# Gated attention and two MLPs on one core: outputs taken transposed, in strips of 32 columns

## What is computed

```python
for t in range(S):                      # a = (a_re, a_im) with its magnitude clamped
    new_re = ar * S_re - ai * S_im
    new_im = ar * S_im + ai * S_re
    kv = np.einsum('bhd,bhe->bhde', k[:, :, t], v[:, :, t])
    S_re, S_im = (new_re + kv, new_im)
    y[:, :, t] = np.einsum('bhd,bhde->bhe', q[:, :, t], S_re)
x = y.transpose(0, 2, 1, 3).reshape(B * S, H * D)      # 3072 x 384
h = x @ w_in;  g = elu(h);  x2 = g @ w_out             # 384 -> 2048 -> 384
out = maximum(x2 @ w1, x2 @ w2, x2 @ w3) @ moe2_w_out  # 384 -> 768 -> 384
```

## Time and profile before

| what | value |
|---|---|
| median of three executions | 1057.25 us (1054.79 to 1057.42) |
| the profiled execution | 1057.7 us, of which the span from the first to the last instruction is 1056.0 us |
| PE busy | 988.4 us, 94% of the span |
| DVE, ACT, POOL busy | 549.1, 439.4, 352.6 us |

### The profile page before, as it was taken

One profiled execution on the slowest core, in us unless ns is written; L12 is line 12 of the kernel. 1 busy time (PEld: TensorE's weight loads), 2 busy tenths in 40 slices (PEclk: granted clock), 3 DMA queues, 4 the chain that ended last, 5 costly groups with the idle time before them and its releaser, 6 DMA issues.

```text
span 1056.0 us, 14734 instructions
## 1 busy us (share of the span) xinstructions
PE 988.4 (94%) x5764; PEld 859.3 (81%) x5764; DVE 549.1 (52%) x720; ACT 439.4 (42%) x669; POOL 352.6 (33%) x277
## 2 busy tenths in 40 slices
PE   3767989989999999999999999999999999999997
PEld 1656879887888888888888788888789898888887
DVE  5888857575868677676858554235331212111110
ACT  5684536354646373736363533234321111212121
POOL 4346432233333343433433322135451212212110
PEclk9778988898999999999999999999999999999999
DMA  6311020202020201011010100140301010100000
GB/s 223 150 46 60 2 76 2 75 1 76 31 76 2 75 32 45 31 46 61 31 46 31 45 17 1 50 175 1 104 1 60 1 60 1 60 8 23 16 16 30
DMA packets 16301, 49.80 MB, mean 47 GB/s; under 512 B 2388, under 2 KB 5460, under 8 KB 15720
## 3 DMA queue, kind: packets, MB, share of 16 engines
q1 hardware_dynamic: 16232, 48.86, 13.4%
HBM read 39.35 MB, written 9.47 MB: 46 GB/s over the span
## 4 chain that ended last, share of the span: by engine, by line
PE 78%; DVE 7%; issue 6%; ACT 3%; POOL 2%; POOLq 0%; DVEq 0%; ACTq 0%
PE bank L997 75%; PE bank L1027 3%; DVE ge L755 1%; DVE t L758 1%; DVE t L780 1%; ACT ge L529 1%; PE bank L1079 1%; POOL hl L418 1%; DVE wil L761 1%; DVE qp L761 1%; DVE ge L758 0%; DVE kp L761 0%; DVE sc L761 0%; DVE xl L761 0%; POOL xl L418 0%
## 5 line engine op out<-in xcount | busy, mean ns | idle before, releaser
L418 POOL TENSOR_TENSOR gl<-ge,gh 128x512 fp32r<-128x512 f32 x96 | 131.4, 1369 | 317.9 <-ACT gh L529 317.9
L761 DVE TENSOR_TENSOR hm<-bank,hm 128x512 f32<-128x512 f32 x72 | 49.8, 692 | 226.6 <-PE bank L997 224.7
L529 ACT ACTIVATE ge<-bank 128x512 f32<-128x512 f32 x96 | 57.1, 595 | 209.5 <-PE bank L997 209.3
L997 PE MATMUL bank<-xh,wih 128*128 128x512 f32 (+1 forms) x336 | 132.4, 394 | 9.4 <-DVE xl L761 9.4
L755 DVE TENSOR_SCALAR ge<-ge 128x512 f32<-128x512 f32 x96 | 55.8, 581 | 157.8 <-ACT ge L529 155.8
L997 PE MATMUL bank<-gh,woh 128*128 128x512 f32 (+1 forms) x336 | 132.1, 393 | 0.7 <-POOL gl L418 0.7
L997 PE MATMUL bank<-xl,wah 128*128 128x512 f32 x324 | 126.3, 390 | 0.0
L997 PE MATMUL bank<-xh,wal 128*128 128x512 f32 x324 | 126.3, 390 | 0.0
L997 PE MATMUL bank<-xh,wah 128*128 128x512 f32 x324 | 126.2, 390 | 0.0
L997 PE MATMUL bank<-xh,wil 128*128 128x512 f32 (+1 forms) x336 | 126.0, 375 | 0.0
L997 PE MATMUL bank<-xl,wih 128*128 128x512 f32 (+1 forms) x336 | 125.7, 374 | 0.0
(11 more groups left out here) (99 smaller groups left out, 2009.9 us busy)
## 6 DMA issues: line engine op xcount, KB each, us to landing
ar<-in_a_re SPq DMA_DIRECT2D x12, 384.0 KB, 3.2
ai<-in_a_im SPq DMA_DIRECT2D x12, 384.0 KB, 3.8
qd<-in_q SPq DMA_DIRECT2D x12, 384.0 KB, 3.7
kd<-in_k SPq DMA_DIRECT2D x12, 384.0 KB, 3.1
vv<-in_v SPq DMA_DIRECT2D x12, 384.0 KB, 3.1
x_rows<-x2s SPq DMA_DIRECT2D x6, 768.0 KB, 3.3
x2r<-x_rows SPq DMA_DIRECT2D x6, 768.0 KB, 6.9
out_x<-osb SPq DMA_DIRECT2D x24, 192.0 KB, 1.9
```

Of the source, the lines that this page charges most:

```text
L418: return nc.gpsimd.tensor_tensor(dst, whole, high.bitcast(f32), ALU.subtract)
L529: return nc.scalar.activation(dst, src, f, **kw)
L761: return nc.vector.tensor_tensor(dst, a, b, op)
L997: return nc.tensor.matmul(dst, lhsT, rhs, start=start, stop=stop)
```

## The change

**Outputs.** `outputs(n)` now does all eight heads in one piece, and makes y transposed, features on partitions. Stationary are 32 columns of the values (or of the state), moving are the 128 columns of the masked scores (or of the transposed q), and the result goes to 32 PSUM partitions. The 384 features are twelve blocks of 32: for each head 32 of its 48 dimensions alone, and the remaining 16 of an even and an odd head together in one block, summed in PSUM with zeros in the gap. That makes 16 products with the scores and, from the second chunk on, 16 more with the state. Four products in a row go to the four strips of 32 partitions.

**What goes.** `y_columns`, `y_rows` and the tile `ysb`; `x_high` and `x_low` read the bank that `outputs` filled. Two pieces fewer take a turn of the three banks (y0, y1, x become y).

**What is laid out anew.** `vv` and `st` have 112 columns for each pair of heads (48, a gap of 16, 48) in place of 96. `increment` writes 64 and 48 columns in turn, `state_add` handles 448 columns in place of 384, and `state_decayed` is two operations on half the heads each. The rows of w_in are permuted on the host in the order of the features.

**The tables.** The last high and low parts of a unit pair stand at place 21, the increment at 22 and the state's addition at 23, so the boundary between tiles (`X_DONE`) comes two places earlier.

```diff
-        vv = sb("vv", [P, PAIR, W], f32, s1)
+        vv = sb("vv", [P, PAIR, H // 2, DP], f32, s1)
...
-        st = sb("st", [D2, B, W], f32, s1)
-        ysb = sb("ysb", [P, W], f32, s1)
+        st = sb("st", [D2, B, H // 2, DP], f32, s1)
...
-        PIECES = [f"{z}_{e}" for z in ("tq", "tk", "s", "lam", "phi", "y0", "y1", "x", "inc") for e in "ab"] + ["halves"]
+        PIECES = [f"{z}_{e}" for z in ("tq", "tk", "s", "lam", "phi", "y", "inc") for e in "ab"] + ["halves"]
...
-            def y_rows(n, half):
-                cols = slice(half * W // 2, (half + 1) * W // 2)
-                src, done = filled(act, f"y{half}", n)
-                if n >= 1:
-                    filled(act, "x", n - 1)
-                func(ysb[:, cols], src[:, cols], ACT.Copy).then_inc(done, 1)
...
-                src, _ = filled(act, "x", n)
+                src, _ = filled(act, "y", n)
...
-                tt(heads(st[:, b, :]), heads(st[:, b, :]), decay[:, b, :].unsqueeze(2).to_broadcast([D2, H, D]),
+                by_pair = decay[:, b, :].rearrange("p (j z) -> p j z", z=2)
+                tt(st[:, b, :, 0:D], st[:, b, :, 0:D], by_pair[:, :, 0:1].to_broadcast([D2, H // 2, D]), ALU.mult)
+                tt(st[:, b, :, DS:DP], st[:, b, :, DS:DP], by_pair[:, :, 1:2].to_broadcast([D2, H // 2, D]),
                    ALU.mult).then_inc(std, 1)
...
-            def outputs(n, half):
+            def outputs(n):
                 e, b, c = n % 2, batch(n), chunk_of(n)
...
-                for h in range(HB * half, HB * half + HB):
-                    cols = slice(h * D, (h + 1) * D)
-                    last = mm(dst[:, cols], sc[:, h, :], vv[:, e, cols], True, c == 0)
-                    if c >= 1:
-                        last = mm(dst[:, cols], qt[:, e, h, :], st[:, b, cols], False, True)
-                last.then_inc(done, 1)
-
-            def y_columns(n):
-                emptied(pe, "y0", n)
-                emptied(pe, "y1", n)
-                dst, done = filling(pe, "x", n)
-                for kk in range(KC):
-                    last = nc.tensor.transpose(dst[:, kk * P:(kk + 1) * P], ysb[:, kk * P:(kk + 1) * P], ident[:, :])
+                emptied(pe, "s0", n)
+                emptied(pe, "s1", n)
+                dst, done = filling(pe, "y", n)
+                state = st[:, b].rearrange("p j d -> p (j d)")
+                for kk, odd, begin, first_, last_ in ((0, 0, 0, True, True), (2, 1, DS + 16, True, True),
+                                                      (1, 0, 32, True, False), (1, 1, D, False, True)):
+                    for old in range(2 if c >= 1 else 1):
+                        for j in range(H // 2):
+                            h = 2 * j + odd
+                            cols = slice(j * DP + begin, j * DP + begin + 32)
+                            start, stop = first_ and old == 0, last_ and (old == 1 or c == 0)
+                            out_ = dst[32 * j:32 * j + 32, kk * P:(kk + 1) * P]
+                            if old:
+                                last = mm(out_, state[:, cols], qt[:, e, h, :], start, stop)
+                            else:
+                                last = mm(out_, values(e)[:, cols], sc[:, h, :], start, stop)
                 last.then_inc(done, 1)
...
-        "x_a": 15, "x_b": 23, "x_high_a": 16, "x_high_b": 23, "x_low_a": 16, "x_low_b": 23,
+        "state_add_b": 23, "x_high_a": 14, "x_high_b": 21, "x_low_a": 14, "x_low_b": 21,
```

More of the change, by code:

```diff
@@ L23, in build @@
     D = 48
+    DS = 64
+    DP = DS + D
     H = W // D
+    WP = H // 2 * DP
     D2 = 2 * D
@@ new lines, in build @@
+        "angle": -8, "halves": -9, "lam_a": -8, "lam_b": -8, "phi_a": -6, "phi_b": -5, "total": -8, "decays_a": -7,
+        "decays_b": -7, "decayed_a": -8, "decayed_b": -6, "reduced_a": -6, "reduced_b": -5, "sines": -4, "rotate_q_a": -3,
+        "rotate_k_a": 0, "rotate_q_b": 3, "rotate_k_b": 7, "tq_a": 1, "tq_b": 6, "tk_a": 2, "tk_b": 12, "s_a": 4, "s_b": 14,
+        "q_evac_a": 1, "q_evac_b": 7, "k_evac_a": 3, "k_evac_b": 12, "masked_a": 4, "masked_b": 15, "state_decay": -3,
+        "state_decayed_a": 6, "state_decayed_b": 12, "y_a": 11, "y_b": 19, "inc_a": 14, "inc_b": 22, "state_add_a": 15,
@@ L59, in build @@
+        "state_add_b": 23, "x_high_a": 14, "x_high_b": 21, "x_low_a": 14, "x_low_b": 21,
     }
     AT_FIRST = {
[L62 removed]
+        "square": -21, "square_im": -21, "squared": -20, "root": -18, "denominator": -17, "ln_first": -17, "ln_second": -15,
         "reciprocal_a": -15, "clamp": -16, "log_decay": -16, "reciprocal_b": -14, "negative": -13, "tangent": -11,
[L64 removed]
+        "arctan": -10, "angle": -9, "halves": -12, "lam_a": -14, "lam_b": -14, "phi_a": -9, "phi_b": -8, "total": -7,
@@ L284, in heads, with pairs @@
             return t.rearrange("p (h d) -> p h d", d=D)
+        def pairs(t):
+            return t.rearrange("p (j d) -> p j d", d=DP)
         def of_set(n):
@@ L366, in _ @@
                     both_parts(u + 1)
[L368 removed]
+            emptied(sp, "y", 2 * NU - 1)
             for n, w in enumerate((w1, w2, w3)):
@@ L1054, in increment, with values @@
                 for h in range(H):
-                    cols = slice(h * D, (h + 1) * D)
-                    last = mm(dst[0:D2, cols], kp[:, e, h].rearrange("p z d -> p (z d)"), vv[:, e, cols], True, True)
+                    cols = slice(h // 2 * DP, h // 2 * DP + DS) if h % 2 == 0 else slice(h // 2 * DP + DS, h // 2 * DP + DP)
+                    last = mm(dst[0:D2, cols], kp[:, e, h].rearrange("p z d -> p (z d)"), values(e)[:, cols], True, True)
                 last.then_inc(done, 1)
-            def outputs(n, half):
+            def values(e):
+                return vv[:, e].rearrange("p j d -> p (j d)")
@@ L1142, in attention @@
                     phase(PAIR * at(x, "phi_b") + 1)
-                if now("y0_a"):
-                    outputs(PAIR * at(x, "y0_a"), 0)
-                if now("y0_b"):
-                    outputs(PAIR * at(x, "y0_b") + 1, 0)
-                if now("y1_a"):
-                    outputs(PAIR * at(x, "y1_a"), 1)
-                if now("y1_b"):
-                    outputs(PAIR * at(x, "y1_b") + 1, 1)
-                if now("x_a"):
-                    y_columns(PAIR * at(x, "x_a"))
-                if now("x_b"):
-                    y_columns(PAIR * at(x, "x_b") + 1)
+                if now("y_a"):
+                    outputs(PAIR * at(x, "y_a"))
+                if now("y_b"):
+                    outputs(PAIR * at(x, "y_b") + 1)
                 if now("inc_a"):
@@ L1234 @@
             a = a.reshape(b, h, s // 128, 128, d).transpose(2, 3, 0, 1, 4).reshape(s // 128, 128, b, h * d)
+        if name == "v":
+            a = a.reshape(*a.shape[:3], h // 2, 2, d)
+            gap = np.zeros((*a.shape[:4], 16), a.dtype)
+            a = np.concatenate([a[..., 0, :], gap, a[..., 1, 32:], a[..., 1, :32]], axis=4).reshape(*a.shape[:3], -1)
         if name == "moe_w_in":
+            f = np.arange(h * d).reshape(h // 2, 2, d)
+            rows = [f[:, 0, :32], np.concatenate([f[:, 0, 32:], f[:, 1, 32:]], axis=1), f[:, 1, :32]]
+            a = a[np.concatenate([z.reshape(-1) for z in rows])]
             a = a.reshape(a.shape[0] // 128, 128, -1, 512).transpose(1, 2, 0, 3)
```

59 lines of the change are left out of this document (19 added, 40 removed).

## The result

The changed kernel is slower: 1094.3 us median of four executions (1090.99 to 1096.11), against 1056.63 us of the kernel before beside it. The ratio is 1.036, with a 95% interval from 1.033 to 1.039. The forecast was 1034 us, faster, with a range up to 1070. Both the sign and the range were wrong.

A forecast was written before the change was run, and what follows sets the result against it. PE's stream was taken as the bound from some 250 us on, DVE up to some 100 us. Terms +5.4 + 0.9 - 9.4 - 12 - 8 = -23.1 us from 1057.7, less 0.45, gave 1034 us; range 1015 to 1070.

The forecast's parts named there:

- DVE, ACT, POOL, SP: Work of these engines: ACT loses 48 copies, a third of their time is free after 250 us; 0 us.
- the chain of one full record for each product: In y, in-order starts let only half of each product overlap: 32 x 107 ns = 3.42 us, about 3.5 with fill.
- The products of y: y in PE's stream: 3.67 us a step against 3.40, +5.4 us; first chunk 1.93 against 1.71, +0.9 us.
- The lower end: Fastest y if all records overlap as far as they can be issued: 64 x 48 ns = 3.07 us.
- Entering the strips: PE's switch to another arrangement of the array ahead of y: 0.17 us, charged once a step.
- The transposes, -9.4 us: Each step loses the transposes ahead of `half_sums` and one more stop of PE: 24 x 0.39 us, -9.4 us.
- The tile boundary, -12 us: At tile boundaries PE's waits for `xl` and the half clock behind them go, 1 us left in all: -12 us.
- The first quarter, -8 us: PE's 6.6 us of early waits for a bank freed by the state's addition go: -8 us, ends 0 and -16.
- the waits move: Rival: boundary and first quarter give nothing, as another piece is late on the three banks; 1054 us, chance 0.09.
- The rival that the strips themselves bring the clock down: Each steady y is followed by 3.4 us of half clock, 1.7 us a step: +34 us, 1068 us, chance 0.07.
- Serial strips: Rival: the strips of y run one after the other, 7.02 us a step; 1104 us, chance 0.20.
- the exposed load: Rival: a product's load can't begin before the preceding matmul starts; y 4.3 to 5.1 us, 1048 to 1064 us, chance 0.12.

The follow-up runs named there:

- e1_early_copies: The changed kernel with the high and low copies of each later unit's first step at place 12, ahead of ACT's sines; 1017.81 us, ratio 0.961 to before.
- e8_q_copy_alone: e1_early_copies with ACT's copy of the second q at place 6, not 7, and the second unit's last high and low copies at 21, not 22; 1010.83 us.
- e7: e1_early_copies with each product of y cut into two of 64 moving columns; 1015.47 us in one execution.
- e3: The kernel before, with ACT's copy of the second half of each unit's first y one place later, behind the sines; 1108.53 us in one execution.
- e2: e1_early_copies with the products of y ordered strip by strip, finishing one strip before the next; 1095.27 us in one execution.
- e4: e1_early_copies with the first unit's first high and low copies at place 6, not 7 and 8; 1019.98 us, ratio 0.965 to before.

## Why the prediction was wrong

Two steps failed, and in opposite directions. The one that turned the sign is the term "DVE, ACT, POOL, SP: nothing": the copy that frees y's bank stood behind ACT's sines, which cost 76.5 us. The other is the chain of one full record for each product, which made y 1.78 us a step too dear. PE's time before, after, and in two of the experiments:

| profiled execution | PE busy | PE idle | span |
|---|---|---|---|
| before | 988.4 us | 67.6 us | 1056.0 us |
| after | 981.5 us | 111.8 us | 1093.3 us |
| e1_early_copies | 943.5 us | 73.1 us | 1016.6 us |
| e8_q_copy_alone | 941.8 us | 69.4 us | 1011.2 us |

**The products of y: wrong by 37 to 39 us, to the good side.** I took 3.67 us a step, and it is 1.89; 20 x 1.78 = 35.6 us. In the first chunk I took 1.93 and 32 records take 1.02 (110.70 to 111.72 in e1), 4 x 0.9 = 3.6 us. The step that failed here is the chain of one full record for each product, "PE starts its matmuls in order": with four strips a product takes half a record of the stream. The lower end was wrong too: I took the 48 ns of `half_sums` as the fastest pace of any record, so that even full overlap gave 3.07 us. A record of 2 moving columns in full-height products one behind another says nothing of records in four strips. I had called these the ends because no row showed two strips at once; with an unseen resource of four parts, a quarter of the serial price, 6.85 / 4 = 1.7 us, belonged in the range.

**Entering the strips: right in kind.** From the end of the last group's turn to y's first record and from y's last turn to the next group there is 0.1 us each, where I charged 0.17 once. The first 0.1 us lies ahead of the 1.89, so a y takes 1.99 us of the stream; counted so, y was too dear by 1.68 us and the term by some 37.

**The transposes, -9.4 us: right as far as the sum shows.** They were not tried apart. In the steady tile of e1, where the late bank is out of the way, y gives 4 x -1.51 and transposes and stops 4 x -0.39, together -7.6 us (-7.2 with the 0.1 us ahead of each y); measured is 112.6 to 105.2, -7.4. Over the whole kernel, y -30.2 and -2.8 in the first chunk, -9.4, and -3.5 for a slightly better clock come to -45.9 us, and PE's busy time fell by 44.9.

**The tile boundary, -12 us: the mechanism held, part of the money went elsewhere.** In after, the wait of the earlier trace rows is gone at the steady boundaries, and the clock stands at 1.00 behind `half_sums` at 439.74. At 251.57 a wait of 1.25 us is left of the 1.90, and at 720.73 there are 1.52 us where I had booked the 1.23 of 681.79 as saved. But as soon as e1 took the big wait away, the 0.36 us for the q copy came up at three `half_sums`, with the half clock behind two of them that I had booked as saved. e8 has that back.

**The first quarter, -8 us: wrong.** The waits on line 858 are gone as I said, but `half_sums` at 51.17 and the scores at 122.16 wait 6.4 us each for `xl`, and the first group of 512 columns starts at 251.57 and not 246.07: +5.5 us. In e1 it starts at 235.71, 10.4 us earlier than before. But y and the transposes alone should give some 12 us up to there (an estimate: 4 x 0.7 + 4 x 1.5 + 8 x 0.39), so nothing shows that the waits of the first quarter gave anything even then. The text had the reason, "a bank's turn may well be late for the next piece instead", and only made the term smaller by it.

**DVE, ACT, POOL, SP: "nothing", and this is the step that turned the sign.** I counted that ACT loses 48 copies and has a third of its time free. What matters is not how full ACT is but what stands ahead of the copy that frees a bank. The last rival, "the waits move", named the right mechanism with 0.09 and 1054 us. Its price was set as the loss of two gains. Its real price is after less e1, 76.5 us: 4.54 us in each of seven units, 3.3 us in two and 2.43 in one, less some 2 us of other waits, and about as much again in half clock.

The number was to be had. y of the first step stands at place 11 and is read at place 14; between them, ACT's queue has the sines with their table loads, 5.3 us (457.20 to 462.49, the same operations as before), and after them a `gh`, a `ge`, the copy and DVE's `xl`. The bank was to be free at the third turn after it, 7 us after y's end. Some 9 to 12 us of hold against 7 us gives a wait of 2 to 5 us in each unit. Before, that bank's first reader stood ahead of the sines. The places 16 and 14 both stood in the change's table. The forecast says nothing of them, and 14 looks like an improvement, being earlier than 16; but at 16 it was the bank of the transposes that waited for `xl`, and y's own bank had been free since 12.

**The clock.** The rival that the strips themselves bring the clock down is refuted: behind the ys at 452.32 in after and at 412.15 in e1 it is 1.00, and e1, with all its strips, has 0.965 against 0.963 before. Serial strips are refuted by y, and so is the exposed load, by e7.

## What to carry to other kernels

When two stages of a ring of buffers are merged into one, write down for each turn when it is filled, which instruction is the last to read it, and what stands ahead of that reader in its own queue. A stage that looked like pure overhead, here the copy to `ysb`, may be what lets the buffer go early. And a stall of PE is to be priced with the slow stretch behind it: here 38.7 us of idle time brought 38.0 us of slower products, and in e3 30.3 us brought 20.5.

## What was not expected of the hardware

- Four strips of 32 columns run side by side in fp32 at 27 ns a record of 128 moving columns and 14 ns a record of 64, against 107 ns for one record alone in the earlier trace rows. Products of different strips need not start in the order of the program (e2, 540.81).
- The turn of an fp32 record in a strip goes by its moving columns: 0.11 us for 128, 0.057 us for 64. With 128 stationary columns it was 107 ns for 48 and for 128 moving columns alike.
- After 4.54 us of idle time the clock was at half for 3.5 to 10 us. After 0.31 to 0.36 us ahead of `half_sums` it was so for some 4 us in three of nine cases (e1, e4, e7) and not at all in the others. The same `half_sums` with no wait ahead of it left the clock at 1.00 (e8).
